# An attention and two feed-forward layers in one kernel: w_in1 turned by VectorE in 32x32 blocks instead of by TensorE

## What is computed

```python
kv_pool = kv.reshape(B, H // 4, 4, W // 4, 4, C).mean(axis=(2, 4))   # 768 keys
k = v = kv_pool.reshape(B, -1, C) @ w_sr
s = (q @ k.T) / sqrt(128); a = exp(s - max(s)); a /= a.sum(-1) + 1e-9
x = a @ v
...
h = x @ w_in1;  g = max(h, 0) + alpha * min(h, 0);  x = g @ w_out1      # d_ff 2048
...
h = x @ w_in2;  P = a0 + a1 h + a2 h^2 + a3 h^3;  Q = 1 + |b0||h| + |b1| h^2
out = (P / (Q + 1e-6)) @ w_out2
```

## Time and profile before

| | |
|---|---|
| median of 3 runs | 1532.26 us (1532.25 to 1532.49) |
| profiled execution: its time | 1533.03 us |
| profiled execution: span of the profile | 1530.6 us, granted clock 0.994 |
| TensorE busy | 1497.5 us (98%) |
| VectorE busy | 1434.1 us (94%) |
| ScalarE busy | 1402.4 us (92%) |
| GpSimd busy | 1259.0 us (82%) |
| DMA on SyncE's and ScalarE's own queues | 23.15 MB |

### The profile page before, as it was taken

The page is one execution under the profiler, slowest core; times in us unless marked ns, Lnnn a source line. Parts: engine busy times, 40 slices in busy tenths (PEclk is TensorE's granted clock), DMA queues, the critical chain, the costliest instruction groups (busy, mean ns, idle before and its releaser), DMA issues. The chain is left out here.

```text
span 1530.6 us, 28132 instructions
## 1 busy us (share of the span) xinstructions
PE 1497.5 (98%) x8181; PEld 1234.5 (81%) x8181; DVE 1434.1 (94%) x2269; ACT 1402.4 (92%) x2714; POOL 1259.0 (82%) x1369
## 2 busy tenths in 40 slices
PE   7999999999999999999999999999999999999986
PEld 6989999768888888888887888887888888888865
DVE  6788888649999999999999999999999999999997
ACT  3787877669999999999999999999999999999996
POOL 1565656329999999999999999999999999999996
PEclk9999999999999999999999999999999999999998
DMA  7211210000000000000000000000000000000000
GB/s 251 55 24 27 51 27 15 1 1 1 8 8 8 1 8 8 8 1 8 8 8 8 1 8 8 8 1 8 8 7 2 7 8 8 8 1 7 8 8 8
DMA packets 62826, 24.94 MB, mean 16 GB/s; under 512 B 48448, under 2 KB 59856, under 8 KB 61904
## 3 DMA queue, kind: packets, MB, share of 16 engines
q1 hardware_dynamic: 62496, 23.08, 6.4%
q10 hardware_dynamic: 176, 0.07, 0.0%
HBM read 16.85 MB, written 6.29 MB: 15 GB/s over the span
## 5 line engine op out<-in xcount | busy, mean ns | idle before, releaser
L321 POOL TENSOR_TENSOR cubic<-sq,lin_p 128x512 f32<-128x512 f32 x384 | 495.5, 1290 | 75.2 <-ACT sq L596 48.3
L312 POOL TENSOR_TENSOR rational<-newton,ratio 128x512 f32<-128x512 f32 x333 | 430.1, 1292 | 30.5 <-PE banks L1616 22.2
L1616 PEld LDWEIGHTS banks<-wout,rational 128*128 128x128 f32 x3072 | 400.8, 193 | 41.9 <-issue 10.6
L1616 PE MATMUL banks<-wout,rational 128*128 128x128 f32 x3072 | 402.9, 276 | 2.5 <-POOL rational L312 1.7
L1396 PE MATMUL banks<-x_hi,win_lo 128*128 128x512 f32 x768 | 386.9, 504 | 15.6 <-DVE ratio L1105 12.3
L1398 PE MATMUL banks<-x_hi,win_hi 128*128 128x512 f32 x768 | 303.8, 396 | 0.0
L1397 PE MATMUL banks<-x_lo,win_hi 128*128 128x512 f32 x768 | 302.9, 394 | 0.0
L614 ACT ACTIVATE lin_p<-banks,ab_raw 128x512 f32<-128x512 f32 x384 | 296.5, 773 | 2.9 <-PE banks L1398 2.8
L1088 DVE SCALAR_TENSOR_TENSOR banks<-sq,abs_b,banks 128x512 f32<-128x512 f32 x384 | 286.2, 746 | 3.3 <-ACT banks L606 2.9
L1105 DVE SCALAR_TENSOR_TENSOR ratio<-banks,ab_raw,rcp 128x512 f32<-128x512 f32 x384 | 285.0, 742 | 3.0 <-POOL rational L312 0.9
L1096 DVE SCALAR_TENSOR_TENSOR banks<-banks,ab_raw,cubic 128x512 f32<-128x512 f32 x384 | 287.6, 749 | 0.0
(11 more groups left out here) (96 smaller groups left out, 2269.2 us busy)
## 6 DMA issues: line engine op xcount, KB each, us to landing
neg_part<-in_q_dram SPq DMA_DIRECT2D x88, 64.0 KB, 2.6
out_dram<-y_out SPq DMA_DIRECT2D x88, 64.0 KB, 2.1
early<-in_kv_dram SPq DMA_DIRECT2D x4, 1024.0 KB, 10.8
early<-in_kv_dram SPq DMA_DIRECT2D x4, 512.0 KB, 9.6
early<-in_moe_w_in_dram SPq DMA_DIRECT2D x1, 1024.0 KB, 17.1
wout<-in_moe_w_in_dram SPq DMA_DIRECT2D x1, 1024.0 KB, 5.2
neg_part<-in_q_dram SPq DMA_DIRECT2D x2, 256.0 KB, 8.8
out_dram<-y_out SPq DMA_DIRECT2D x2, 256.0 KB, 2.2
```

Source lines behind the costliest of these rows:

```text
L312: nc.gpsimd.tensor_tensor(rational[:, m % 3, :], newton[:, m % 2, :], ratio[:, m % 2, :], ALU.mult).then_inc(s["rat_done"], 1)
L321: nc.gpsimd.tensor_tensor(cubic[:, m % 2, :], sq[:, m % 2, :], lin_p[:, m % 2, :], ALU.mult).then_inc(s["cubic_done"], 1)
L1616: last = nc.tensor.matmul(banks[:, ACC2, t * P:(t + 1) * P], rational[:, m % 3, t * P:(t + 1) * P], wout2[:, c, :], start=(c == 0 and t == ...
```

## The change

w_in1 is loaded a second time, into a free area of `early` (`swapped_in1`), by sixteen DMAs of 64 KB with runs of 128 bytes, in which the 32x32 blocks are already in their exchanged places; j and r are the block's column and row within a 128x128 block. VectorE turns the blocks with four transposes (`turn_in1` on VectorE), two behind the maximum of tile 3 of step 0 and two behind the reciprocal after it. The identity products and the evictions are gone. In SyncE's queue w_out1 now comes first after kv, then the sixteen loads, then w_in1 itself, then the coefficients and the queries as before. The wait for `v_lo_done` moves from the first identity product to the first turned probabilities in step 1.

```diff
+        swapped_in1 = early[:, tokens // 2 + 2 * ff:tokens // 2 + 3 * ff].rearrange("p (b r c) -> p b r c", b=BLOCKS, c=SIDE)
...
+            sp.dma_start(wout1[:], w_out1.rearrange("(b p) c -> p b c", p=P)).then_inc(s["ld_out1"], 16)
+            in1_parts = w_in1.rearrange("(r a) (b j c) -> j r a b c", a=SIDE, b=BLOCKS, c=SIDE)
+            for j in range(P // SIDE):
+                for r in range(P // SIDE):
+                    sp.dma_start(swapped_in1[j * SIDE:(j + 1) * SIDE, :, r, :], in1_parts[j, r]).then_inc(s["ld_swapped"], 16)
             sp.dma_start(raw_in[0], w_in1).then_inc(s["ld_in1"], 16)
-            sp.dma_start(wout1[:], w_out1.rearrange("(b p) c -> p b c", p=P)).then_inc(s["ld_out1"], 16)
...
-            def in1_transposed(n):
-                act.wait_ge(s["in1_t_ready"], n + 1)
-                nc.scalar.activation(w_in1_t[:, 4 * n:4 * n + 4, :].rearrange("p b c -> p (b c)"), banks[:, TURNED[n], :],
-                                     ACT.Copy).then_inc(s["in1_t_done"], 1)
...
+            def turn_in1(n):
+                dve.wait_ge(s["ld_swapped"], 16 * (P // SIDE) ** 2)
+                nc.vector.transpose(w_in1_t[:, 4 * n:4 * n + 4, :], swapped_in1[:, 4 * n:4 * n + 4, :, :]).then_inc(s["in1_t_done"], 1)
...
                 maxima(g, 3)
+                if g == 0:
+                    turn_in1(0)
+                    turn_in1(1)
                 inverse(g, 2)
+                if g == 0:
+                    turn_in1(2)
+                    turn_in1(3)
...
-            def turn_in1(n):
-                pe.wait_ge(s["ld_in1"], 16)
-                pe.wait_ge(s["v_lo_done"], 2)
-                after(pe, s["in1_t_done"], n - 1)
-                for j in range(4):
-                    c = 4 * n + j
-                    last = nc.tensor.transpose(banks[:, TURNED[n], j * P:(j + 1) * P], raw_in[0][:, c * P:(c + 1) * P], ident[:])
-                last.then_inc(s["in1_t_ready"], 1)
...
                     if g == 0 and c == 0:
-                        pe.wait_ge(s["in1_t_done"], 4)
+                        pe.wait_ge(s["v_lo_done"], 2)
```

## The result

The changed kernel takes 1536.04 us (median of 13 runs, 1533.52 to 1537.58) against 1532.57 for the kernel before (13 runs beside it, 1529.18 to 1535.29): the ratio is 1.0020, with a 95% interval of 1.0012 to 1.0027. That is +3.5 us, more than twice the +1.6 that were forecast, and 0.2 us inside the range. The profiled execution took 1537.18 us, with a span of 1535.0.

A forecast was written before the change was run, and what follows sets the result against it. TensorE was taken to bound the kernel, in an unbroken run from 35.25 us. Removed 0, added the longer of 0.9 (transposes) and 1.6 us (late queries), on a median of 1532.3: 1533.9 us, range 1532.4 to 1536.2.

The forecast's parts named there:

- the late queries: Step 1: third group's query loads, queued behind the added loads, hold the query transpose and later scores; delay 1.6 us.
- rival (b): SyncE's queue: scattered loads issue slower, 1537.7 us, or the queue is released no earlier, 1536.4 us; chance 0.12.
- Removed work is worth nothing: Steps 0 and 1: identity products and evictions lie off the chain; removal worth 0 to 0.07 us, taken as 0.
- First term: Step 1: four VectorE transposes end at 37.2 us and delay the linear weight's first products, +0.9 us.
- Release of SyncE's queue: SyncE's queue, with w_in1 no longer ahead of w_out1, lets the sixteen loads issue from 20.4 us instead of 22.87.
- Coefficients: SyncE's queue: two coefficient loads ahead of the queries, between 0.43 and 1.19 us each, 1.6 us taken for both.
- Landing of the queries: Third group's fourth query load, issued at 35.7 us, lands 2.7 us later, at 38.4.
- X: Time at which the third group's fourth query load lands: 38.4 us, ends 37.2 and 39.3.
- Zero of the sum: Step 1 scores that started at 39.89 us before: delay is the queries' landing time minus 36.76, 1.6 us.
- Rival (c): TensorE's clock falls after pauses of 1.4 and 2.0 us in steps 0 and 1; about 3 us more, 1537; chance 0.03.
- The Trainium skill's two rules: TensorE advised for 128x128 transposes, trace agreeing; DMA initiation usually small, trace disagreeing: 128-byte-run loads issue every 0.68 us.

The follow-up runs named there:

- the second profile of before: Kernel before the change, unaltered, run and profiled once more: 1532.70 us, ratio 1.0001 to the kernel before.
- The kernel with w_in1 behind: Changed kernel with only the plain w_in1 load issued behind the query loads, coefficient loads still ahead: 1534.66 us, ratio 1.0014 to the kernel before.
- the loads alone: Kernel before plus the sixteen small loads behind w_in1 and w_out1, read by nobody: 1538.75 us, ratio 1.0036.
- the three busy ones: Sixteen unread identity products added to: changed kernel, 1537.09 us; it with w_in1 and coefficients behind queries, 1532.58; that with linear weight waiting per part, 1533.07.
- waits by part and TensorE kept busy: Changed kernel, w_in1 and coefficients behind queries, each linear-weight part waiting only for transposes it reads, sixteen unread identity products: 1533.07 us, ratio 1.0001.
- the changed kernel again: Changed kernel, unaltered, run and profiled once more: 1535.38 us, ratio 1.0015 to the kernel before.

## Why the prediction was right, and where it was off

Forecast were 1533.9 us in a range of 1532.4 to 1536.2; measured were 1536.04. Sign, place and mechanism were as said: the late queries set the delay. Its size was not: +3.5 us by the medians, +3.3 by the trace, against +1.6. The term that was mis-sized is the time from issue to landing of the query loads (2.7 us taken, 4.5 measured). That the time still lies in the range, by 0.2 us, is partly luck: the forecast itself was given for delays of 0.9 to 3.0 us, and the range reached further only to take in the lower edge of rival (b), whose causes were not the ones at work. Point by point:

- *Removed work is worth nothing.* Right. The first scores of step 1 stand 8.43 us after S, against 8.40 before.
- *First term, four transposes in front of the linear weight, +0.9.* Right in kind; 0.6 to 0.9 in size where it was alone. A pair takes 1.3 us (1.31 and 1.28 in the timeline above), not 1.4.
- *Release of SyncE's queue.* Forecast 20.4 us, measured 19.74; the second profile of before lets the queue go at 22.17 where the first has 22.87, so the forecast fits an execution that begins as early as this one. The reason given, that enough of w_out1 must be fetched, stays unproven: the queue went on 0.2 us before the load ahead of w_out1 had landed in the kernel before (w_in1, 23.09) and 0.15 before it in the changed one (the last of kv, 19.89), while w_out1 landed at 27.05 and 23.79. The next loads then went slower than 0.68 us (one took 1.67, at 22.45), so the last one issued at 30.87, forecast 30.6. They landed at about 33.85, forecast 33.6, and VectorE waited 0.32 us for them, forecast none; by the prediction's own list that wait is a sign of (b), though a small one. The 0.7 us of room was spent by an early execution, in which VectorE came to them at 33.57.
- *Coefficients.* 1.6 us was forecast for both, and they took 0.43 each, the lower end. The queries therefore issued at 33.15, ahead of the 33.7 forecast, and the fourth at 35.09, ahead of 35.7.
- *Landing of the queries.* This is the term that was mis-sized: 2.7 us from issue to landing, the median of all such loads, where 4.5 was measured. That median is over 88 loads, most of which have no large load right in front. I had w_in1's megabyte in the upper end of X (39.3) and not in the value taken. X came out at 39.54 (the transpose's start at 39.59, less 0.05). The kernel with w_in1 behind shows what the megabyte did: 2.3 us without it.
- *Zero of the sum.* I set X against 39.89, a time of an execution that began late by 0.7 us. With S at 26.21, as in the changed kernel's profile, these scores would have stood at 26.21 + 13.05 = 39.26 without the change, so the delay is X - 36.13, and X = 39.54 gives 3.4. By X - 36.76 it would be 2.8. Of the 1.7 us between forecast (+1.6) and T (+3.3), 1.1 is X and 0.6 is this, less 0.1, as the chain from X to the scores took 3.00 us and not 3.13. The landing moves less than the start: the query's transpose began at 39.45, 39.59 and 39.69 with S at 26.07, 26.21 and 26.45.
- *Rival (b), the small loads are slow.* Not so, or hardly: the last of the sixteen was issued within 0.3 us of the forecast. But the release came 0.7 us earlier than forecast, so they took 0.9 us more between the two.
- *Rival (c), the clock.* I gave it 0.03, and its sign, a granted clock under 1.00 in 30 to 50 us, appeared. It fell in one of the two profiles of the changed kernel and, over all kernels without products in the two places, in five of eight; in the six with products there (the two of before, the loads alone, and the three busy ones) it never fell between 34 and 41 us. My ground against it was that the kernel before paused for 1.14 us at full clock. That says nothing of the pauses of 1.4 and 2.0 us that the rival itself foresaw, and they came as 1.37 and 2.06. Five of eight against none of six is suggestive, not proof. The price of 3 us had no row behind it; 1.55 was measured where nothing hid the fall. That it cost the changed kernel little is owed to the late queries, which covered it.
- *The Trainium skill's two rules.* "VectorE: DVE Perf Modes", section "Rules for kernel authors", to turn 128x128 on TensorE where PSUM will do, held here as far as no form with VectorE's transposes was faster: with its data there and one wait for all four it costs 0.6 us, and with waits by part and TensorE kept busy it comes out level (13.05, 1533.07 us). "DMA: Bandwidth & Descriptors" in the Trainium skill, section "Issuing engines are not separate DMA queues", that the time to initiate a DMA is usually small beside it, holds for one such load (0.63 us of issue, 2.5 to 3.0 to its landing, from 24.84 on), but a row of them is bound by it: they issue back to back at 0.67 us each from 24 to 31 us while the engines stand at a share of 0.57 to 0.72 (26 to 31 us).

The profiled execution of the changed kernel ends 4.4 us of span later than that of before, more than the 2.8 us by which its Y is later. The last stretch, from 1473 to 1496 us on by profile, has pieces at the lower clock in every profile, and how many fall before the end differs from run to run; I read no cause of the change in it.

## What to carry to other kernels

Read what stands idle beside the work that you remove: here TensorE's identity products lay in gaps, so that nothing came back, and they also kept its pauses short. Before you put loads into a queue, follow each transfer behind them to the instruction that needs it, and price its landing with the bytes that are in front of it, not with its usual latency; a large load that nobody needs yet goes behind the small one that is due. Measure shifts from an event inside the run (here the first scores), as a start that varies by 0.9 us blurs an effect of 3.

## What the hardware showed beyond expectation

- TensorE's granted clock fell to the 1.2 GHz level in some executions of the same program and not in others, after pauses of 1.4 and 2.0 us; after pauses of 0.5 and 1.2 us it was not seen to fall. A pause of 2.20 us ahead of 42.64 (the changed kernel again) was not followed by a fall, while within pauses of 2.49 and 3.68 us in the same place the clock fell. Where nothing else was late, one such fall cost 1.55 us (14.60 against 13.05); after the pause of 3.68 us a longer one cost 2.4 us.
- Of four DMAs of 64 KB the last landed 2.3 us after its issue with w_in1 behind them, and 4.5 us with its 1 MB in front.
- Between w_in1's data and the queries' data the 16 DMA engines were nearly idle (a share of 0.20 and 0.35 in 36 to 38 us, with the query loads issued from 33.15 on). With the coefficient loads elsewhere the hole was gone, but the fourth query load was issued no sooner and landed no sooner. What holds that issue and that landing is open.
